# Token groups of 448, 448, 448, 448 and 320 columns, and a load ring of four, in a Strassen-like token-mixing kernel

## The reference

```python
theta = x @ w_theta
zr, zi = x * np.cos(theta), x * np.sin(theta)
y = einsum('ts,bsd->btd', w_tok_r, zr) + einsum('ts,bsd->btd', w_tok_i, zi)
u = x + y
x = u + np.maximum(u @ w_ch, 0.0)
# then: h = x^T @ U @ V;  u = x + h^T;  out = u + np.maximum(u @ w_ch1, 0.0) @ w_ch2
```

## Time and profile before

| | |
|---|---|
| median of 3 runs | 2867.97 us (2867.37 to 2873.16) |
| the profiled execution: time / span | 2859.61 us / 2857.8 us |
| busy: PE, PEld, DVE, ACT, POOL | 96%, 93%, 76%, 35%, 8% |
| granted TensorE clock, mean | 0.987 |
| HBM traffic | 139 GB/s mean |
| loads of w_raw by SP, sums by POOL | 220 and 220, 636 KB each, median 3.9 and 6.2 us to landing |

### The profile page before, as it was taken

The page is one execution under the profiler, slowest core; times in us unless marked ns, Lnnn a source line. Parts: engine busy times, 40 slices in busy tenths (PEclk is TensorE's granted clock), DMA queues, the critical chain, the costliest instruction groups (busy, mean ns, idle before and its releaser), DMA issues.

```text
span 2857.8 us, 37049 instructions
## 1 busy us (share of the span) xinstructions
PE 2740.8 (96%) x14491; PEld 2645.9 (93%) x14491; DVE 2174.3 (76%) x2498; ACT 1009.2 (35%) x1349; POOL 219.4 (8%) x252
## 2 busy tenths in 40 slices
PE   2799999999999999999999999999999999999999
PEld 2789999999999999999999999999999998999999
DVE  7778878878877888789788888887766875665665
ACT  3233333333333333333333333333322443343443
POOL 3000100101001001001010010010110000000000
PEclk7999999999999999999999999999999999999999
DMA  6656766757767668677677686685773000010000
GB/s 179 149 135 191 179 159 190 169 169 177 182 178 194 145 189 187 163 188 163 179 174 177 181 192 147 189 187 155 183 179 101 33 1 21 27 37 29 27 29 34
DMA packets 102782, 397.87 MB, mean 139 GB/s; under 512 B 10704, under 2 KB 28784, under 8 KB 102512
## 3 DMA queue, kind: packets, MB, share of 16 engines
q0 software_dynamic: 31680, 143.29, 28.1%
q1 hardware_dynamic: 70960, 252.60, 25.1%
HBM read 356.92 MB, written 38.93 MB: 139 GB/s over the span
## 4 chain that ended last, share of the span: by engine, by line
PE 62%; DVE 22%; issue 8%; DMA 5%; ACT 3%; SPq 0%; DVEq 0%; ACTq 0%
PE bank L1010 13%; PE bank L1011 13%; PE bank L1009 13%; DVE attn L657 7%; DMA z_raw<-z_out 4%; DVE w_l L713 2%; PE bank L1101 2%; PE bank L1104 2%; PE bank L1105 2%; PE bank L1103 2%; PE bank L1102 2%; DVE z_op L708 2%; DVE Y L736 2%; PE bank L979 1%; PE bank L1089 1%
## 5 line engine op out<-in xcount | busy, mean ns | idle before, releaser
L1009 PE MATMUL bank<-w_h,z_op 128*128 128x424 f32 (+1 forms) x3465 | 1235.1, 356 | 27.9 <-DVE zf L703 17.8
L1010 PE MATMUL bank<-w_l,z_op 128*128 128x424 f32 (+1 forms) x3465 | 1231.3, 355 | 0.0
L1011 PE MATMUL bank<-w_h,z_op 128*128 128x424 f32 (+1 forms) x3465 | 1230.3, 355 | 0.0
L438 ACT ACTIVATE w_h<-w_raw 128x1272 fp32r<-128x1272 f32 x385 | 487.0, 1265 | 1122.5 <-PE bank L1011 1048.1
L1009 PEld LDWEIGHTS bank<-w_h,z_op 128*128 128x128 f32 x3465 | 653.0, 188 | 46.6 <-DVE zf L703 18.0
L1010 PEld LDWEIGHTS bank<-w_l,z_op 128*128 128x128 f32 x3465 | 652.8, 188 | 17.2
L1011 PEld LDWEIGHTS bank<-w_h,z_op 128*128 128x128 f32 x3465 | 652.4, 188 | 16.0
L713 DVE TENSOR_TENSOR w_l<-w_raw,w_h 128x1272 fp32r<-128x1272 f32 x385 | 569.1, 1478 | 60.6 <-ACT w_h L438 60.5
L410 POOL DMA_DIRECT2D w_raw<-in_w_tok x220 | 193.4, 935 | 1942.2 <-DVE w_l L713 1406.9
L917 DVE SCALAR_TENSOR_TENSOR hid_l<-bank,hid_h 128x384 fp32r<-128x384 f32 x264 | 144.4, 557 | 149.5 <-ACT hid_h L601 146.1
L743 DVE TENSOR_TENSOR Y<-Y,bank 128x1272 f32<-128x1272 f32 (+1 forms) x110 | 162.0, 1472 | 102.3 <-PE bank L1011 70.9
(11 more groups left out here) (114 smaller groups left out, 3054.4 us busy)
## 6 DMA issues: line engine op xcount, KB each, us to landing
w_raw<-in_w_tok SPq DMA_DIRECT2D x220, 636.0 KB, 3.9
w_raw<-in_w_tok POOLq DMA_DIRECT2D x220, 636.0 KB, 6.2
z_raw<-z_out SPq DMA_DIRECT2D x88, 576.0 KB, 6.5
z_out<-zf SPq DMA_DIRECT2D x66, 384.0 KB, 5.4
x_win<-in_xin SPq DMA_DIRECT2D x22, 585.0 KB, 5.8
out<-res SPq DMA_DIRECT2D x22, 576.0 KB, 2.8
v_raw<-in_v SPq DMA_DIRECT2D x11, 144.0 KB, 2.6
w_raw<-in_w SPq DMA_DIRECT2D x1, 1536.0 KB, 6.7
```

What stands on the lines that cost most here:

```text
L438: nc.scalar.activation(w_h[:, s % WRING], w_raw[:, SLOT[s]], ACT.Copy).then_inc(wh_ready, 1)
L1009: mm(o, zh, wh, start=(k == 0 and not goes_on), stop=False, skip_group_check=goes_on)
L1010: mm(o, zh, wl, start=False, stop=False, skip_group_check=goes_on)
L1011: last = mm(o, zl, wh, start=False, stop=(k == KC - 1), skip_group_check=goes_on)
```

## The change

`TW` becomes 448, so that the groups are 448, 448, 448, 448 and 320 wide, still 2112 in sum. The ring of loads has four slots in place of five. `w_hi` and `w_lo` work on the `width(g)` columns of the group and not on all TW. The transfers still move 128 x (3 x TW), padding included.

```diff
-TW = 424
+TW = 448
...
-RAWS = 5
+RAWS = 4
...
-                nc.scalar.activation(w_h[:, s % WRING], w_raw[:, SLOT[s]], ACT.Copy).then_inc(wh_ready, 1)
+                n = width(STAGES[s][2])
+                nc.scalar.activation(w_h[:, s % WRING, :, 0:n], w_raw[:, SLOT[s], :, 0:n], ACT.Copy).then_inc(wh_ready, 1)
...
-                vec.tensor_tensor(w_l[:, s % WRING], w_raw[:, SLOT[s]], w_h[:, s % WRING].bitcast(F32),
-                                  ALU.subtract).then_inc(wl_ready, 1)
+                n = width(STAGES[s][2])
+                vec.tensor_tensor(w_l[:, s % WRING, :, 0:n], w_raw[:, SLOT[s], :, 0:n],
+                                  w_h[:, s % WRING, :, 0:n].bitcast(F32), ALU.subtract).then_inc(wl_ready, 1)
```

## The result

The changed kernel took 2856.91 us (median of 6 runs, 2855.01 to 2858.67) beside 2870.88 us for the kernel before (6 runs, 2867.37 to 2877.97): a ratio of 0.9948, 95% interval 0.9933 to 0.9963. The change makes the kernel faster by 8 to 14 us. I had forecast no change, at 2870 us.

What follows compares the result with a forecast made beforehand. PE, busy 96% of the span, was taken as the bound, with waits for DVE's convolution before theta. Terms -4.5 + 5.5 + 0 + 1 = +2 us on the median of 2867.97 gave 2870 us, range 2855 to 2896.

Steps and rivals of the forecast that it cites:

- the term 0 for the rate of PE: PE's matmuls: cost taken as a line in the columns, four wide stages at +0.27 us and a narrow at -1.08, sum 0.
- The sign that the prediction itself had named: PE's stages: the forecast is wrong if wide and narrow ones don't make 5.49 x 4 + 4.02 us.
- The three sizes that lay within 3 ns of a line: Matmul spacings at 384, 416 and 424 columns, the evidence for taking the middle, 0, within the bounds.
- The bound of 17 us either way: PE's rate: mixing slopes of 0.5 and 0.417 ns per column for wide and narrow gives +17 or -17 us.
- the spacing isn't a line: Rival on PE's matmuls: address or length acts on spacing, up to 17 us; chance 0.15 for gain, 0.07 for loss over 6.
- The wait ahead of stage 31: PE's wait for DVE before theta: falls to 1.6 us, 0.5 less, nine times, -4.5 us.
- ACT's delay: Turn 25: DVE stood still 0.76 us for ACT's sines; about 0.46 goes; if it stayed, the wait is 2.05 us.
- The wait ahead of stage 13: PE's wait for DVE before theta: grows to 1.66 us, 0.6 more, nine times, +5.5 us.
- 0.33 us of handing over: Ahead of stage 13: added to DVE's 14.89 us for turns 10 to 12 to get the wait of 1.66 us.
- The transfers: Loads and sums with the shorter ring: only stage 10 is tight, w_hi late by 0 to 1 us; +1 us.
- The rival of the ring: Stage 10: its sum takes 12.5 us, so w_hi comes late; 26 us slower, 2894 us; chance 0.12.
- The floor of the narrow matmul: Rival at 320 columns: weight loads keep spacing above 149 ns, up to 173.5; up to +51 us, 2919 us; chance 0.12.

Runs made afterwards that it cites:

- e3: Kernel before with the seventh tap of each convolution one turn earlier on DVE; 2828.56 us, ratio 0.9863.
- e4: Changed kernel with the seventh tap of each convolution one turn earlier on DVE; 2818.56 us, ratio 0.9833.
- e1: Kernel before with a ring of four load slots and nothing else changed; 2864.39 us, ratio 0.9982.
- e6: Changed kernel with groups of 464 columns four times and 256, rows 464 columns apart; 2871.16 us, ratio 1.0012.
- e8: Changed kernel with w_hi and w_lo over all 448 columns for the narrow group too; 2888.12 us, ratio 1.0077.
- second pair: Profiles of the repeats of both kernels, e7 for before and e12 for after; main parts 2173.2 and 2164.7 us.
- second series: Changed kernel timed again, later, beside the kernel before; 2862.32 us beside 2870.14 us, ratio 0.9973.
- e7: Kernel before once more, unchanged, a single run for a second profile; 2866.55 us.
- e2: Kernel before with a ring of four and rows of w_h and w_l 448 columns apart; 2861.30 us, ratio 0.9978.
- e14: Kernel before's widths (424 and 416), ring of four, rows in SBUF and DRAM 448 columns apart; 2873.64 us, ratio 1.0013.
- e9: Changed kernel with groups of 416 columns four times and a last one of 448, rows 448 apart; 2879.89 us, ratio 1.0030.
- e15: Kernel before with POOL's memset of Y held back until the first three taps are done; 2871.63 us, ratio 0.9996.
- e12: Changed kernel once more, unchanged, timed beside the others; 2862.32 us, ratio 0.9973.
- e13: Changed kernel's widths (448 and 320) with rows in SBUF and DRAM 456 columns apart; 2868.57 us, ratio 0.9988.

## Why the prediction was wrong

**The step that failed** is the term 0 for the rate of PE: "the change is free on PE exactly if the cost of a matmul is a line in its columns". It isn't one, in this kernel. The term measured -10 to -11 us (set 962.3 to 957.4; e3 to e4 -10.0 us in the time). The sign that the prediction itself had named shows it: five stages take 957.4 x 27 = 25.85 us in place of 4 x 5.49 + 4.02 = 25.98, so 77 times 0.13 us less. The three sizes that lay within 3 ns of a line hid it, since one ns in each matmul is already 10 us. The bound of 17 us either way held, and the rival *the spacing isn't a line* had the right mechanism, as far as it goes (address or length act on the spacing), down to its evidence, the stages of one width between 5.19 and 5.24 us. I gave its gain 0.15. That observation wanted a number: the three slots of before run at 192.3, 193.4 and 194.2 ns, a spread of 2 ns in a term of which 1 ns is 10 us.

**The wait ahead of stage 31** was sized at 1.6 us and -4.5 us. It is 2.06 in eight places and 0.58 in the first, against 2.18 and 1.19: -1.6 us. ACT's delay stayed, at 0.60 us of 0.76, and the text's own sentence for that case had 2.05. The step that failed is that the longer stage 24 and the shorter turn 24 would take 0.46 us off this delay; they took 0.16, and DVE's turns 25 to 30 need 33.05 us and not 32.73.

**The wait ahead of stage 13** was right in its mechanism and nearly in its size: 14.89 us forecast for DVE's turns 10 to 12 and 14.90 measured, a wait of 1.66 forecast and 1.85 to 1.86 measured in eight of nine places (2.26 in the ninth). A part of this is PE's three stages, which were shorter still than by the line, and a part a slip in the sum: its 0.33 us of handing over gives 15.84 + 0.33 - 15.45 = 0.72 us for the case before, where rows 4 have 0.81. In sum the wait costs +7.6 us in the first pair of profiles and +4.6 in the second, in place of +5.5.

**The transfers** were forecast at +1 and cost nothing: sum of stage 10 at 1116 forecast, 1115.00 measured; w_hi not late. The rival of the ring fell with e1.

**The floor of the narrow matmul** doesn't exist down to 256 columns: 146.5 ns at 320, 118.2 at 256 in e6. Weight loads recorded with 189 ns follow each other every 146.5 ns, so they overlap, and PEld's busy time falls from 2645.9 to 2563.2 us for it. The nine transposes held against this rival start 109 ns apart and not 100; the 0.90 us has in it a last distance of 0.03 us to a matmul of another kind.

**What no term had:** the clock. Behind a wait of about 2 us ahead of theta it sometimes falls, for 1.4 to 1.8 us each. It struck 2 of 18 times in both first profiles, and so cost no difference here, but e8 shows it as some 13 of the 24 us by which its profile is longer than that of after.

By these terms the sum is -10.3 - 1.6 + 7.6 + 0 = -4 us in the first pair of profiles and -10.8 - 1.6 + 4.6 = -8 in the second, beside -3 and -8 us in their main parts, -14 in the first series of timed runs and -8 in the second. That the median still lies in the range of 2855 to 2896, 2 us above its lower end, is no merit of the sum. Three of the first series' six runs of before lay at 2873 to 2878, against 2867.4 to 2868.6 for the others, with none of the kind in the six of after; without them the difference is 11 us. The second pair agrees with the second series; between the first pair and the first series 10 us are left, or 7 without those three runs, and they stay open: more falls of the clock in timed runs of before than in its profile would do it, and e7's four falls point that way, but no timed run has a trace.

## What to carry to other kernels

When a change keeps the columns of the matmuls and moves only where they are cut, the rate needn't be constant: measure the start-to-start spacing to 0.1 ns, stage by stage, leave out the stages behind a pause or another block, and where stages of one shape differ by the slot that they read, try other row pitches and widths before trusting a line. A gain of rate is kept only where PE isn't waiting for another engine in the same stretch; here one tap moved by one turn was worth 30 to 40 us, three times the change. And where groups get unequal, every helper that works on a group has to shrink with the small one: without the slices this change would have been a loss.

## What the runs showed of the hardware

- A matmul's spacing depends on where its moving operand lies: with rows 448 columns apart in place of 424 (e1 to e2) 416 columns take 186.9 ns in place of 189.3, and 424 take 193.3 in all three slots in place of 191.9, 193.4 and 193.7.
- At one width, pitch and stage number it can have several levels: 190.0 and 193.4 ns at 424 columns in e14.
- Behind a theta block the first distance from start to start in a stage is 266 ns, against 191 else (before and after).
- Over the columns' own time at 2.4 GHz a matmul of the stages costs 11.5 ns at 256 columns, 13.2 at 320, 16.0 at 448 and 16.6 at 424 and pitch 424. The Trainium skill, TensorE: Matmul & The Clock Gate, section Wait — 56ns, not 53.3ns?, has a fixed 2.5 ns for its case; this pattern, where each matmul has new weights, is far from that and not fixed, and here the measurement decides.
- The granted clock fell to 1.2 GHz behind idle times of PE of 2.07 us (in after, at 1445) and 2.65 us (in e8, at 964), for 1.4 to 1.8 us of loss, in 19 profiles behind none of 118 waits of up to 1.85 us and 53 of 151 longer ones.
- A TENSOR_SCALAR of DVE can stand until a row of 24 memsets on POOL is over: 21.3 us for one instruction in e9, 12.9 in e15, 10.0 in e12 and e13; in the 15 other profiles none took over 1.8 us.
